# Weight pieces loaded raw into the place of their low parts, keys and queries requested by ScalarE, the threshold moved to VectorE

## What is computed

```
# attention: 4 batches x 8 heads, 576 tokens, head size 64
scores = (q @ k.T) / 8
thresh = max(scores, row) - tau
attn   = exp(where(scores >= thresh, scores, -1e9) - max); attn /= sum(attn) + 1e-9
x      = attn @ v                      # -> 2304 tokens x 512
# first feed-forward: d_ff 2048
h = x @ w_in;  g = max(h, 0) + alpha * min(h, 0);  y = g @ w_out
# second: gated product, then two matrices
out = ((y @ w1) * (y @ w2)) @ w3 @ w_out2
```

## Time and profile before

| | us |
|---|---|
| median of 3 runs | 1081.94 (1080.91 to 1084.33) |
| the profiled execution, time | 1082.92 |
| its span, first to last instruction | 1081.0 |
| TensorE busy | 999.7, 92% of the span |
| VectorE, GpSimd, ScalarE busy | 498.0, 473.1, 446.9 |
| step 64 (start of the interleaved chunks) | at 180.2 |
| last attention tile | at about 460 |
| chunks 6 and 7 alone | 504.1 to 561.5 |
| eight chunks with w_b, then last stage | 561.5 to 769.9, 769.9 to 1077.3 |

### The profile page before, as it was taken

How to read it: one execution, slowest core, us unless ns; L and a number is a source line. 1 busy time by engine, 2 the same in 40 slices (tenths; PEclk the granted TensorE clock), 3 DMA queues, 4 the chain that set the end, 5 groups by cost and what they waited for, 6 DMA issues and landing times.

```text
span 1081.0 us, 18083 instructions
## 1 busy us (share of the span) xinstructions
PE 999.7 (92%) x6848; PEld 910.5 (84%) x6848; DVE 498.0 (46%) x1224; ACT 446.9 (41%) x1146; POOL 473.1 (44%) x586
## 2 busy tenths in 40 slices
PE   3699867889899897999999999999999999999998
PEld 2577645777778686879999999999999999999998
DVE  4798976878878786931322222222111111111111
ACT  6677665756656665532333333333112111111211
POOL 5877677846555664421334444444212112111211
PEclk9999966999999999999999999999999999999999
DMA  5599988587877767474442334347211011011000
GB/s 175 149 252 269 265 236 273 155 241 177 238 181 187 220 159 218 114 219 151 145 158 72 137 138 155 135 152 281 89 58 42 34 67 45 22 67 45 23 22 23
DMA packets 51623, 156.38 MB, mean 145 GB/s; under 512 B 8144, under 2 KB 19408, under 8 KB 47312
## 3 DMA queue, kind: packets, MB, share of 16 engines
q1 hardware_dynamic: 45008, 141.07, 42.2%
q10 hardware_dynamic: 6528, 14.16, 5.4%
HBM read 80.22 MB, written 32.51 MB: 104 GB/s over the span
## 4 chain that ended last, share of the span: by engine, by line
PE 57%; DVE 11%; DMA 9%; SPq 7%; ACT 7%; POOL 5%; issue 3%; ACTq 1%; POOLq 0%
PE psum L631 19%; PE psum L663 19%; PE psum L617 10%; DVE nmx L859 4%; DMA xy<-xs 3%; PE psum L577 3%; SPq L397 3%; DVE e_ring L866 3%; PE psum L542 2%; POOL g L970 2%; SPq L400 2%; ACT e_ring L731 2%; DVE g_raw L898 2%; PE psum L590 1%; DMA xs<-x_hl 1%
## 5 line engine op out<-in xcount | busy, mean ns | idle before, releaser
L970 POOL TENSOR_TENSOR g<-g_raw,g 128x288 fp32r<-128x288 f32 x192 | 157.7, 825 | 372.1 <-ACT g L844 235.1
L663 PE MATMUL psum<-xy,w_a 128*128 128x288 f32 x1536 | 206.1, 295 | 0.6 <-DVE y_buf L954 0.6
L663 PEld LDWEIGHTS psum<-xy,w_a 128*128 128x128 f32 x1536 | 205.1, 188 | 0.8 <-DVE y_buf L954 0.8
L525 PE MATMUL psum<-ks,qs 128*128 128x288 f32 x640 | 124.1, 325 | 45.8 <-DVE e_ring L866 29.7
L525 PEld LDWEIGHTS psum<-ks,qs 128*128 128x128 f32 x640 | 104.3, 210 | 60.8 <-DVE e_ring L866 35.5
L1004 POOL TENSOR_SCALAR e_ring<-e_ring,rden,uni 128x576 f32<-128x576 f32 x144 | 118.6, 825 | 60.6 <-DVE rden L877 58.5
L866 DVE SCALAR_TENSOR_TENSOR e_ring<-psum,thr,e_ring 128x576 f32<-128x576 f32 x144 | 117.5, 816 | 40.4 <-ACT e_ring L731 39.7
L841 ACT COPY g_raw<-psum 128x288 f32<-128x288 f32 x64 | 25.6, 400 | 236.2 <-PE psum L663 236.2
L898 DVE SCALAR_TENSOR_TENSOR g_raw<-g_raw,beta_sb,psum 128x288 f32<-128x288 f32 x128 | 65.2, 514 | 125.3 <-ACT g_raw L765 124.8
L859 DVE TENSOR_REDUCE nmx<-psum 128x1 f32<-128x576 f32 x144 | 108.5, 753 | 29.1 <-PE psum L525 28.9
L577 PEld LDWEIGHTS psum<-xy,w_a 128*128 128x128 f32 x576 | 80.7, 192 | 45.7 <-DMA xy<-xs 19.2
(11 more groups left out here) (54 smaller groups left out, 1124.8 us busy)
## 6 DMA issues: line engine op xcount, KB each, us to landing
xy<-xs SPq DMA_DIRECT2D x16, 1152.0 KB, 6.2
zbuf<-ybuf SPq DMA_DIRECT2D x96, 180.0 KB, 3.9
zbuf<-ybuf SPq DMA_DIRECT2D x96, 144.0 KB, 4.2
raw_w<-weights SPq DMA_DIRECT2D x52, 256.0 KB, 4.0
k_raw<-k SPq DMA_DIRECT2D x16, 576.0 KB, 6.1
q_raw<-q SPq DMA_DIRECT2D x16, 576.0 KB, 7.0
xs<-x_hl SPq DMA_DIRECT2D x32, 288.0 KB, 4.7
ys<-xy SPq DMA_DIRECT2D x8, 1152.0 KB, 4.4
```

The source lines that it names most:

```text
L525: last = mm(dst, qs[:, par, at:at + P], ks[:, par, part, h, cols], start=(m == 0), stop=(m == 2 * len(terms) - 1))
L663: last = mm(psum[:, 2 * ab + f % 2, 0:CH], w_a[:, wp, slot, (f % 4) * P:(f % 4 + 1) * P], xy[c][:, xp, kt, :], start=(n == 0), stop=(n == ...
L970: sub = lambda out_, a, hi: nc.gpsimd.tensor_tensor(out_, a, hi.bitcast(F32), ALU.subtract)
```

## The change

- Piece j of `w_a` and `w_b` is loaded raw into the slot where its low part will stand (`raw_a`, `raw_b` are the same memory seen as float32), cast from there, and the low part overwrites it. The four small raw buffers are gone. Pieces 0 to 15 are requested at once at the start, later ones two steps ahead of their cast (`load_piece`).
- New tables: casts of pieces 0 to 9 in steps 2 to 11, 10 to 23 in every second step from 13 to 39, 24 to 39 in steps 45 to 63. The products run in steps 12 to 43 instead of 18 to 49. VectorE subtracts pieces 1, 3, 5 and 7 and, as before, half of the later ones.
- Keys and queries are requested on ScalarE's queue (steps 9n+4 and 9n+8). Those of pair 0 are split in another order, all low parts on VectorE, and the scores start when four low parts are made.
- The x of a batch's last pair goes straight to the even chunk that needs it (`s_xd`); the other three quarters of that chunk are loaded eight steps ahead. Odd chunks are loaded whole, eight steps ahead.
- The 16 pieces of the second half are requested at once when attention's memory is free, and the last 16 at once after chunk 7.
- The threshold is made on VectorE behind the maximum. Where a hidden unit ends with three or more units left in its step (f = 3 and 4 of a chunk), its activation is made in the same step instead of the next.

```diff
-Q_STEPS = {2: 0, 4: 1}
+FIRST_HI = [0, 2, 1, 3, 4, 5]
+FIRST_LO = [0, 1, 4, 5, 2, 3, 6, 7, 8, 9]
+FIRST_KEYS = 6
...
-PIECE_STEPS = [3, 4] + list(range(9, 15)) + [15 + 4 * i + m for i in range(FT) for m in range(2)]
-PIECE_STEPS += list(range(52, 52 + N_M1))
-PRODUCT_STEPS = [18 + 4 * i + a for i in range(FT) for a in range(4)]
+PIECE_STEPS = list(range(2, 12)) + [9 + 4 * i + 2 * m for i in range(1, FT) for m in range(2)]
+PIECE_STEPS += [45 + 6 * i // 5 for i in range(N_M1)]
+PRODUCT_STEPS = [12 + 4 * i + a for i in range(FT) for a in range(4)]
...
-            def load_early(j):
-                if j >= 4:
-                    sp.wait_ge(s_w_lo[j % 2], (j - 4) // 2 + 1)
-                sp.dma_start(early_raw(j), weights[j]).then_inc(s_e_in[j % 4], 16)
...
+            def load_piece(j):
+
+                slot = early_slot(j)
+                if N_WP <= j < EARLY:
+                    sp.wait_ge(s_wp, FT)
+                elif 2 * FT <= j < N_WP:
+                    sp.wait_ge(s_wp, (j - 2 * FT) // 2 + 1)
+                sp.dma_start(raw_a[:, 1, slot, :], weights[j]).then_inc(s_w_in[slot], 16)
...
             def load_interleaved(ck):
+
                 if ck >= 1:
                     sp.wait_ge(s_h, FT * ck)
-                sp.wait_ge(s_xs, 32 * PAIRS * (ck // 2 + 1))
-                sp.dma_start(xy[0][:, :, :, :].bitcast(F32), xs[ck]).then_inc(s_xa_in, 16)
+                if ck % 2 == 0:
+                    sp.wait_ge(s_xs, xs_stored(PAIRS * (ck // 2) + PAIRS - 1))
+                    sp.dma_start(xy[0][:, :, 0:PAIRS - 1, :].bitcast(F32), xs[ck, :, :, 0:PAIRS - 1, :])\
+                        .then_inc(s_xa_in, 16)
+                else:
+                    sp.wait_ge(s_xs, xs_stored(PAIRS * (ck // 2 + 1)))
+                    sp.dma_start(xy[0][:, :, :, :].bitcast(F32), xs[ck]).then_inc(s_xa_in, 16)
...
+                if kt == PAIRS - 1:
+                    if b >= 1:
+                        sp.wait_ge(s_h, FT * 2 * b)
+                    sp.dma_start(xy[0][:, :, kt, :].bitcast(F32), x_hl[:, :, 0:CH].bitcast(F32)).then_inc(s_xd, 16)
...
-                    for j in range(4):
-                        load_early(j)
-                if pair_at(s, 5) is not None and pair_at(s, 5) + 1 < NPAIR:
-                    load_keys(pair_at(s, 5) + 1)
-                if pair_at(s, 8) is not None and pair_at(s, 8) + 1 < NPAIR:
-                    load_queries(pair_at(s, 8) + 1)
+                    for j in range(2 * FT):
+                        load_piece(j)
+                for j in range(2 * FT, EARLY):
+                    if s == PIECE_STEPS[j] - 2:
+                        load_piece(j)
...
-                if piece_at(s) is not None and 4 <= piece_at(s) + 3 < EARLY:
-                    load_early(piece_at(s) + 3)
...
-                if fill(s + 4) is not None and fill(s + 4)[1] == 0:
-                    load_interleaved(fill(s + 4)[0])
+                if fill(s + 8) is not None and fill(s + 8)[1] == 0:
+                    load_interleaved(fill(s + 8)[0])
...
+            for slot in range(SLOTS):
+                load_b_piece(slot)
...
+            act.dma_start(q_raw[:, :, :], q[0]).then_inc(s_q_in, 16)
...
+            def load_keys(n):
+                if n == 1:
+                    act.wait_ge(s_kq_first, FIRST_KEYS)
+                else:
+                    act.wait_ge(s_kq_lo, kq_lo_made(n - 1, 4))
+                act.dma_start(k_raw[:, :, :], k[n]).then_inc(s_k_in, 16)
...
-            def threshold_of(t):
+            def exp_of(t):
                 i = t % TILES
                 act.wait_ge(s_max, t + 1)
...
+                for ck, f in hidden_early(s):
+                    negative_of(ck, f, fbank(f))
...
+                if s % TILES == 4 and s // TILES + 1 < NPAIR:
+                    load_keys(s // TILES + 1)
+                if s % TILES == 8 and s // TILES + 1 < NPAIR:
+                    load_queries(s // TILES + 1)
...
+            def threshold_of(t):
+                i = t % TILES
+                dve.wait_ge(s_max, t + 1)
+                nc.vector.tensor_scalar(thr[:, i:i + 1], nmx[:, i:i + 1], tau_sb[:, 0:1], None, ALU.add)\
+                    .then_inc(s_thr, 1)
```

More of the change, by code:

```diff
@@ L115, in units_at, with hidden_ends, hidden_early, hidden_late @@
     return [(at[0], *u) for u in UNITS_AT[at[1]]] if at else []
+def hidden_ends(s):
+    units = units_at(s)
+    return [(ck, f, len(units) - 1 - at) for at, (ck, kind, f, i) in enumerate(units) if kind == "h" and i == KD - 1]
+def hidden_early(s):
+    return [(ck, f) for ck, f, left in hidden_ends(s) if left >= 3]
+def hidden_late(s):
+    return [(ck, f) for ck, f, left in hidden_ends(s) if left < 3]
 def hidden_done(s):
-    return [(ck, f) for ck, kind, f, i in units_at(s) if kind == "h" and i == KD - 1]
+    return [(ck, f) for ck, f, left in hidden_ends(s)]
+def xs_stored(n):
+    return 32 * n
 def y_done(s):
     return [(ck, m) for ck, kind, m, i in units_at(s) if kind == "y" and i == FT - 1]
-def piece_at(s):
-    return PIECE_STEPS.index(s) if s in PIECE_STEPS else None
+def pieces_at(s):
+    return [j for j, at in enumerate(PIECE_STEPS) if at == s]
+def by_vector(j):
+    return j % 2 == 1 and (j < FT or j >= EARLY)
+def lo_counts(n):
+    by = sum(by_vector(j) for j in range(n))
+    return n - by, by
+def loads_into(j):
+    return sum(early_slot(i) == early_slot(j) for i in range(j + 1))
 def product_at(s):
@@ L195, in sem @@
             return ctx.enter_context(nc.semaphore(name))
+        with ExitStack() as place:
+            raw_a = sb("raw_a", [2, SLOTS, PC], F32, place)
         w_a = sb("w_a", [2, SLOTS, PC], F32R)
-        raw_w = sb("raw_w", [2, PC])
         alpha_sb = sb("alpha_sb", [FF1 // P])
@@ L224, in build @@
         attn.close()
+        with ExitStack() as place:
+            raw_b = sb("raw_b", [2, SLOTS, PC], F32, place)
         w_b = sb("w_b", [2, SLOTS, PC], F32R)
@@ L257, in build @@
         s_xs = sem("x_stored")
[L259 to L260 removed]
+        s_w_in = [sem(f"weight_piece_loaded_{i}") for i in range(SLOTS)]
+        s_b_in = [sem(f"second_half_piece_loaded_{i}") for i in range(SLOTS)]
         s_w_hi = sem("weight_hi_made")
@@ L478, in _ @@
             sp.wait_ge(s_yp_out, 16 * 2 + 16)
+            for j in range(EARLY + N_M1, EARLY + 2 * N_M1):
+                load_piece(j)
             for ck in range(NCH):
@@ L547, in split_pieces @@
             def split_pieces(n):
-                for par in range(2):
-                    pe.wait_ge(s_w_lo[par], n // 2)
+                for by in range(2):
+                    pe.wait_ge(s_w_lo[by], lo_counts(n)[by])
             def unit(ck, kind, x, a):
@@ L781, in _ @@
                         x_hi(pair_at(s, LAG_X[part // 2]), part)
-                if piece_at(s) is not None:
-                    early_hi(piece_at(s))
+                for j in pieces_at(s):
+                    early_hi(j)
                 if product_made(s - 1) is not None:
@@ L804, in _ @@
                 n, parts = parts_at(s, HI_STEPS, HI_PARTS)
-                for part in parts:
-                    if n == 0 and part in (2, 3):
-                        scale_q(n, part - 2)
+                for part in FIRST_HI if n == 0 and parts else parts:
                     split_kq_hi(n, part)
@@ L924, in _ @@
                     reciprocal_of(tile_at(s, 1))
+                for ck, f in hidden_early(s):
+                    activation_of(ck, f, 0, fbank(f))
+                for j in pieces_at(s):
+                    if by_vector(j):
+                        early_lo(j)
                 for part in range(X_PARTS):
```

179 lines of the change are left out of this document (90 added, 89 removed).

## The result

The changed kernel takes 1091.5 us (median of 11, 1087.4 to 1096.8) against 1084.27 for the kernel before on the same chip (11 runs, 1080.87 to 1086.49): ratio 1.0074, 95% interval 1.0053 to 1.0096. It is 0.7% slower. I had forecast 1054.6, a range of 1032 to 1072, and 0.91 for faster: wrong, and outside the range on the far side.

The account below looks back on a forecast made before the run. TensorE, busy 92% of the span, bounds the kernel except up to step 64, where the row maxima set the pace. Terms -27.4 - 5.0 - 2.7 + 7.8 = -27.3 us give 1054.6 us, range 1032 to 1072.

Parts of the forecast that it names:

- Steps 21 to 64: The 43 steps before the chunks: 138.7 us against 130.9, 7.8 lost, as pieces land late behind block moves.
- The seven named waits: ScalarE's waits for pieces cast in steps 25, 35, 45, 51, 52, 60 and 61: 29.9 us in all.
- the 4 us "that TensorE gets ahead": Steps 21 to 64: TensorE gets ahead in the first two piece waits and hides 4 us of its own excess.
- Keys and queries compete with the moves: Rival, chance 0.22: keys requested amid block moves make seven late pieces some 1.7 us later each, 12 us, 1066.6.
- The chunks, 27.4: Interleaved chunks: 27.4 us won, from 16.4 of load waits, 8.5 of clock and 2.5 of activation and threshold.
- The clock term of 8.5: Chunks: TensorE's low clock behind the load waits costs 1.7 us a chunk, five times, 8.5 us won.
- The activation's 0.5 a chunk: Chunks: early hidden activation, with the threshold, wins 0.5 us a chunk, 2.5 in all.
- Start, 2.7 won: Steps 9 to 21: 2.7 us won as GpSimd's overload goes; step 9 comes at some 15.7.
- Chunks 6 and 7, 5.0 won: Second halves of chunks 6 and 7: requesting all 16 pieces at once removes waits, 5.0 us won.
- Threshold, 1.2 won: Threshold on VectorE: 0.08 us off some 15 steps before step 64, 1.2 us won.
- The pieces are not late: Rival, chance 0.18: shorter moves or earlier piece requests make the 29.9 less 4 us vanish, 1028.7.
- Slower: loads land late: Rival, chance 0.07: seven pieces and the queries of pairs 2 to 6 land late, 41.7 us, 1096.3.

Follow-up runs that it names:

- run 1: The changed kernel with pieces 16 to 39 requested eight steps ahead of their cast instead of two: 1070.82 us, 0.9878 of the kernel before.
- Run 2: The changed kernel with keys and queries requested on SP's queue, pieces still two steps ahead: 1092.79 us, 1.0078 of the kernel before.
- Run 10: The kernel before with keys and queries requested on ScalarE's queue and nothing else: 1091.25 us, 1.0058 of the kernel before.
- run 5: The kernel before with only the straight chunk load, requested eight steps ahead: 1073.79 us, 0.9882 of the kernel before.
- run 4: The changed kernel with every hidden activation made in the next step, as before: 1088.09 us, 1.0043 of the kernel before.
- run 15: Run 9 with every hidden activation made in the next step: 1060.62 us, 0.9794 of the kernel before.
- run 8: Run 1 with keys and queries requested on SP's queue: 1064.53 us, 0.9801 of the kernel before.
- run 16: Run 13 with the first piece cast in step 3, behind pair 0's keys and queries: 1053.46 us, 0.9719 of the kernel before.
- run 13: Run 12 with pieces 1, 3, 5, 7 back on VectorE, GpSimd first waiting for ten low parts: 1054.96 us, 0.9724 of the kernel before.
- Run 12: Run 9 with pieces 1, 3, 5, 7 on GpSimd, pieces 8 to 23 cast earlier, no early activation: 1056.98 us, 0.9727 of the kernel before.
- 9: Run 8 with pieces 24 to 39 cast in steps 52 to 67: 1061.83 us, 0.9780 of the kernel before.
- run 6: The kernel before with the threshold on VectorE and nothing else: 1082.40 us, 0.9971 of the kernel before.

## Why the prediction was wrong, point by point

- **Steps 21 to 64** is the step that failed most: 7.8 lost was forecast, 22.1 came. The mechanism, a piece behind twelve moves with two steps of lead, was right and run 1 shows it. Its size was not: the term that failed is the landing of 4.3 us that all seven waits were worked out with. The seven named waits measured 38.0 for 29.9 (cast 25: 6.7 for 5.3; 45: 7.0 for 2.0; 51: 4.0 for 2.2; the others within 1.3), and one was missed (step 33, 6.9), which with 4.3 us would have been 1.4. With the 44.9 measured in place of 29.9 the sum gives 153.7 for the 43 steps, and 153.0 came: the other terms, the 4 us "that TensorE gets ahead" among them, held together. The eight pieces took 6.9 us to land. The 4.3 was a median of the whole program, in which 32 of the 52 loads of `raw_w` come later and take 3.0; between steps 21 and 64 the trace of before itself has

```profile
raw_e<-weights SPq DMA_DIRECT2D x12, 256.0 KB, 5.5
raw_w<-weights SPq DMA_DIRECT2D x12, 256.0 KB, 6.7
```

So the right size could be read before the change was run.
- **Keys and queries compete with the moves**, my rival at 0.22 and +12 us: it was at work together with the forecast, and I had put it only on the pieces. (Its sum had a slip: a third of 6.1 us is 2.0, not 1.7, so 14 us and not 12.) Run 2 shows that for the pieces it goes both ways: two of them wait less with the keys moved, those behind a whole burst more. Run 10 measures it alone at +0.6% and shows where it goes: to the store of x and the block moves, and into the chunks, which the prediction had left out of it. The rule that I had cited from the Trainium skill, "DMA: Bandwidth & Descriptors", section "Issuing engines are not separate DMA queues", that another issuer brings no other DMA engines, fits this part. Of what I took for its contrary, the issue time of the moves, 1.5 us up to step 44 was real. The Trainium skill, "DMA: Bandwidth & Descriptors", section "Queues, rings and completion order", adds that an engine goes in turns between the queues that have work; the landing of the store of x, 4.7 against 6.2 us, fits it.
- **The chunks, 27.4.** 15.1 came. "I take all of the 16.4 us" failed: the load waits stood over waits on the activation (run 5: 14.5 away, 8.1 back). The clock term of 8.5 gave 6.1 in run 5; in the changed kernel busy time fell by only 2.7, and the early activation accounts for a part (without it 1.8 less in run 4, 4.3 less in run 15). The activation's 0.5 a chunk had the wrong sign in the traces. New small waits came: 3.1 for moves, which go with the keys on ScalarE's queue (run 8 has none), and 4.0 for ScalarE's copies of y, which need that and the early activation together (1.3 in run 8, 0.4 in run 4).
- **Start, 2.7 won:** 3.0 lost. I counted three pieces ahead of the first maximum, 15.7; it came at 18.9. Two other things cost: the keys' cast stood behind piece 0, a wait of 5.7 us (run 16: keys 2.8 us sooner), and the subtractions on VectorE took four times as long beside GpSimd's (4.21 against 1.04 us for four, run 13). From step 12 to 21 the 2.7 were not won either: step 12 is 3.1 us late and step 21 3.0. TensorE waits 5.9 of its 7.8 us for low parts of pieces there, since the products moved six steps ahead and GpSimd's work did not keep up. Run 12, which casts those pieces sooner, brings step 21 forward by 6.1 us, the largest gain at the start.
- **Chunks 6 and 7, 5.0 won:** 2.2 in the profiled execution, 3.8 to 4.0 in those of runs 1, 8, 9 and 16. The waits for pieces are gone, but loads that are all requested at once were not free: ScalarE waits 2.6 to 2.8 us for a store of y beside them in all of these. **Threshold, 1.2 won** with 0.5 a chunk: run 6 measures 0.3%, about 3 us (interval 0.9 to 5.3), with step 64 1.7 us sooner: right.
- **Rivals.** "The pieces are not late" is out. "Slower: loads land late" had the right sign at 0.07. It wanted a mean landing of 8.3 us and more (7.9, if its two terms are added); the mean was 6.9, and the loss came from one more late piece, the start, the keys and the smaller gain. The chances were too sharp for a sum in which a gain of 27 us stood on hidden waits that no row had excluded.

The time forecast, 1054.6, is about that of run 13 (1055.0). That is chance and bears nothing out: run 13 has eight steps of lead, keys on SP's queue, later casts of pieces 24 to 39, an earlier and reordered start and no early activation, and it still wins less in the chunks than was forecast.

## What to carry to other kernels

Before booking a wait as won, list the waits that end within a microsecond or two of it on the same engine; they are what is late next, and here they gave back more than half. When a request moves to another queue, count what stood ahead of it in the old queue as now sharing with it, and look for who waits for that. And give a prefetch a lead in steps that covers the longest burst of its queue, not its median landing; where a landing time is needed, read it in the stretch in question and not over the whole program (6.7 against 4.0 us here).

## What the runs showed of the hardware that I had not expected

VectorE and GpSimd slow each other in subtractions of two SBUF operands. Four query subtractions on VectorE take 1.04 us with GpSimd idle, 4.21 with it busy for most, 5.21 for all of the time; a 128x16 instruction takes 0.17 or 1.14; a 128x512 piece 0.68 or 1.67, while GpSimd's own takes 1.28 or 1.57. The Trainium skill, "SBUF — State Buffer", section "SBUF: two separate sides", states that the two share one port pair, held by one instruction at a time. The traces agree in the main: 5.21 us for four is 1.30 each, about the 1.28 that one piece takes on GpSimd, and a piece on VectorE takes 0.68 us at least and 1.28 in the median of the changed kernel. But a pair of pieces, one on each engine, takes 1.67 us in run 13, less than the 0.68 and 1.28 together, so not all of an instruction's time is exclusive. The prediction had used 0.97 us a piece from the earlier trace rows, a mean that lies between the two cases.

A store of 288 KB lands in 4.5 to 4.9 us (median) in every run with key loads in its own queue and in 5.6 to 6.6 in every run with them in the other one.
